# Sparse attention and a rational MLP on one core: the tensor between them stays on chip, turned, and the order of all instructions comes from a table

## The chip, the cores and the metric

One core of a Trainium2 chip runs the whole program in one launch. The metric is device time in microseconds (us). The engines are TensorE (PE in the rows, with its weight loads as PEld), VectorE (DVE), ScalarE (ACT), GpSimd (POOL) and SyncE (SP); here the last two only issue DMAs. Each engine works through its own list in order and waits on semaphores.

## The reference

Attention over 8 batches x 8 heads x 576 tokens x 64 dimensions, then an MLP over the 4608 tokens:

```
scores = q @ k.T / 8
heads 0-3 (local):   key j is seen by query i if 0 <= i-j < 32
heads 4-7 (strided): key j is seen by query i if j <= i and j % 32 == i % 32
x = softmax(masked scores) @ v          -> [4608, 512]
h = x @ w_in                            (512 -> 2048)
P = a0 + a1 h + a2 h^2 + a3 h^3
Q = 1 + |b0| |h| + |b1| h^2
out = (P / (Q + 1e-6)) @ w_out          (2048 -> 512), float32
```

The MLP needs x turned: its 512 features on the partitions, the tokens along the row.

## The kernel before

**Attention, batch by batch.** POOL issues DMAs that cast q, k, v from float32 to bf16: into DRAM scratch (`qk16`, `v16`) for batches 2 to 7, and, for batches 0 and 1, q and k into SBUF staging tiles `sg` (L441). SP then loads: for batches 2 to 7 three DMA transposes bring q and k with the head dimension on the partitions (`sqkT` L485, `lqT` and `lkT` L491); for batches 0 and 1 TensorE turns `sg` (L537) and DVE and ACT write the result out of PSUM (L553), `lqT` and `lkT` with a stride of 8 elements on the written side. The local V goes from the bf16 scratch into `vL` in 128-byte rows (L500, L508 for batches 0 and 1; L500, and L514 for the shifted copy, after that). `vS` (strided V) is cast straight into SBUF by POOL (L454).

Scores are small matmuls into PSUM (L599, L614 strided; L674 local) on top of a mask matmul (L586, L660). A row maximum (DVE L631, L698) is subtracted by a matmul (L638, L705), and ACT takes the exponential (L644, L711, L715) into `pS` and `pL`. P is turned: by TensorE and an eviction for batches 0 and 1 (L571, L578), by a DMA transpose on SP after that (L561). For the strided heads a matmul with `BO` gives the row sums (L734), DVE inverts them (L738); P is stationary and V moves (L750), two PSUM tiles of two banks one after the other, each scaled by DVE into `xS` (L757). For the local heads a column of ones in `vL` gives the sum beside P.V (L783, three banks), DVE scales into `xl` (L800, L803).

**x goes through DRAM.** `xS` and `xl` are stored in token order to `xs16` by SP: four DMAs (L765), one (L808) and two (L817) per batch. One or two DMA transposes per batch (L870, the function `gather`) bring x back turned into `xt`, a ring of three tiles of 512 tokens. For chunk 0's 512 tokens (batch 0) and the last 448 tokens of chunk 1 (batch 1) `turn_x` does it on TensorE (L836, L853) with evictions L843 and L860.

**The MLP, in 9 chunks of 512 tokens.** 16 groups of four matmuls (L889) make h in PSUM; ACT writes each out (L893). Then per group of 2 to 8 blocks of 512: |h| on ACT (L909; on DVE for chunk 0, L913), Q on DVE (L916, L918), 1/Q as exp(-ln Q) on ACT (L922, L927), P on DVE (L931 to L939), the product (L941). L957 multiplies by w_out, ACT evicts (L965), SP stores (L971).

**What sets the order.** `Prog.schedule` (L124) is a list planner: each operation carries an assumed duration and a key, `_place` (L113) gives PSUM banks (8 in all) as they come free in the plan, and the result is one fixed list per engine. `emit` (L219) adds the semaphore waits. Attention of batch b+1 is laid among the MLP of chunk b. The casts of batch b+2 wait until the loads of batch b+1 have landed.

Of the kernel before, what the change touches and what calls it, by code (L numbers as in the profile page):

```python
# [12 lines left out]
NBANK = 8  # L13
# [9 lines left out]
class Op:  # L23


    def __init__(self, eng, maker, dur, occ, key, dma, bank):
        self.eng, self.maker, self.dur, self.occ, self.key = eng, maker, dur, occ, key
        self.dma, self.bank = dma, bank
        self.dst = None
        self.gen = 0  # L30
        self.deps = {}
        self.users = []
        self.fin = None


class Tile:
# [9 lines left out]
    def new(self):  # L46
        self.prev = self.w + self.r
        self.w, self.r = [], []
        self.gen += 1
        return self  # L50


class Banks:

    def __init__(self, n):
        self.n = n
        self.ops = []
        self.w, self.r, self.prev = [], [], []  # L60
        self.at = None
        self.left = 0

    def col(self, bank=0, c=0):
        return (self.at + bank) * 512 + c


class Prog:
    ENG = ("pe", "act", "dve", "pool", "sp")

    def __init__(self, nc):
        self.nc = nc
        self.ops = []

    def op(self, eng, maker, dur, key, r=(), w=(), m=(), dma=None, occ=None, after=(), hard=()):
        bank = None
        for t in tuple(w) + tuple(m):
            if isinstance(t, Banks) and not t.ops:
                bank = t
        o = Op(eng, maker, dur, dur if occ is None else occ, key, dma, bank)  # L80
# [12 lines left out]
        o.hard = hard  # L93
# [6 lines left out]
        for t in tuple(r) + tuple(w) + tuple(m):  # L100
            if isinstance(t, Banks) and o not in t.ops:
                t.ops.append(o)
        o.banks = [t for t in dict.fromkeys(tuple(r) + tuple(w) + tuple(m)) if isinstance(t, Banks)]
        if dma is not None:
# [7 lines left out]

    def _place(self, n, t):  # L113
        rng = range(0, NBANK - n + 1) if n > 1 else range(NBANK - 1, -1, -1)
        best = None
        for i in rng:
            f = max(self.bfree[i:i + n])
            if f <= t:
                return i, f
            if best is None or f < best[1]:  # L120
                best = (i, f)
        return best

    def schedule(self):  # L124
        E = self.ENG
        for o in self.ops:
            o.ndep = len(o.deps)
            o.ready = 0.0
            for d in o.deps:
                d.users.append(o)  # L130
            for b in o.banks:
                b.left += 1
        self.bfree = [0.0] * NBANK
        self.blast = [[] for _ in range(NBANK)]
        ready = {e: [] for e in E}
        free = {e: 0.0 for e in E}
        order = {e: [] for e in E}
        qfree = {'hw': 0.0, 'sw': 0.0}
        for o in self.ops:
            if o.ndep == 0:  # L140
                ready[o.eng].append(o)
        left = len(self.ops)
        while left:
            best = None
            for e in E:
                q = ready[e]
                if not q:
                    continue
                t0 = free[e]
                pick = None  # L150
                block = False
                soon = None
                for o in sorted(q, key=lambda o: (o.key, o.idx)):
                    s = max(t0, o.ready)
                    if o.bank is not None:
                        if block:
                            continue
                        at, f = self._place(o.bank.n, s)
                        if f > s + 1e-9:
                            s = f  # L160
                            if o.bank.n > 1 and o.ready <= t0 + 1e-9:
                                block = True
                    if s <= t0 + 1e-9:
                        pick = (t0, o)
                        break
                    if s < 1e8 and (soon is None or s < soon[0] - 1e-9):
                        soon = (s, o)
                c = pick or soon
                if c is not None and (best is None or c[0] < best[0] - 1e-9):
                    best = (c[0], e, c[1])  # L170
            assert best is not None, "no bank"
            t, e, o = best
            if o.bank is not None:
                b = o.bank
                at, f = self._place(b.n, t)
                assert f <= t + 1e-6
                b.at = at
                for i in range(at, at + b.n):
                    for d in self.blast[i]:
                        o.deps.setdefault(d, 1)  # L180
                    self.bfree[i] = 1e9
            ready[e].remove(o)
            free[e] = t + o.occ
            o.start = t
            if o.dma is not None:
                us, lat = o.dma
                me, other = ("sw", "hw") if o.eng == "pool" else ("hw", "sw")
                s = max(qfree[me], t + o.dur)
                rest = max(0.0, qfree[other] - s)
                if us <= rest:  # L190
                    qfree[me] = s + 2 * us
                    qfree[other] += us
                else:
                    qfree[me] = s + us + rest
                    qfree[other] += rest
                o.fin = qfree[me] + lat
            else:
                o.fin = t + o.dur
            order[e].append(o)
            left -= 1  # L200
            for b in o.banks:
                b.left -= 1
                if b.left == 0:
                    end = [x for x in b.ops]
                    f = max(x.fin for x in end) + 0.1
                    for i in range(b.at, b.at + b.n):
                        self.blast[i] = end
                        self.bfree[i] = f
            for u in o.users:
                lat = (0.15 if o in u.hard else 0.035) if u.eng == o.eng else 0.1  # L210
                u.ready = max(u.ready, o.fin + lat)
                u.ndep -= 1
                if u.ndep == 0:
                    ready[u.eng].append(u)
        self.order = order
        self.span = max(o.fin for o in self.ops)


    def emit(self):  # L219
        nc = self.nc  # L220
        sems = {e: nc.alloc_semaphore(f"s_{e}") for e in self.ENG}
        cnt = {e: 0 for e in self.ENG}
# [15 lines left out]
        for o in self.ops:  # L238
            if o.dma is not None:
                semof[src(o)] = o.dst.sem  # L240
# [69 lines left out]
def bass_strided_sparse_attn__then__act_rational_pade_kernel(nc, q, k, v, moe_w_in, moe_w_out, moe_a, moe_b, out):  # L310
# [7 lines left out]
    CH = 512  # L318
# [725 lines left out]
```

How the kernel before makes its waits and increments, by code:

```python
            def go(eng):  # L279
                for ws, o in queues[e]:
                    for s, n in ws:
                        eng.wait_ge(s, n)
                    inst = o.maker(eng)
                    if o.dma is not None:
                        inst.then_inc(o.dst.sem, 16)
                    else:
                        inst.then_inc(sems[e], 1)
                if e == "sp":
                    for s, n in fin.items():
                        eng.wait_ge(s, n)
```

## Time and profile before

| | us |
|---|---|
| median of 3 runs | 450.33 (449.14 to 452.17) |
| span of the profiled execution, first to last instruction | 441.2 |
| what lies around the span: median less span | 9.1 |
| PE busy / DVE busy / ACT busy | 339.6 / 331.8 / 323.4 |
| DMA, hardware queue (SP) / software queue (POOL), share of 16 engines' span | 47.0% / 25.4% |
| mean granted TensorE clock (1 is 2.4 GHz) | 0.919 |

The page gives the profiled execution by its span alone, so sums are made against 441.2 us, and 9.1 us are added to compare with the runs. Three engines are each busy for about three quarters of the span: the rows have to say what they wait for, and when.

### The profile page before, as it was taken

To read this page: it belongs to the slowest core of one execution; us is meant where nothing else is said; L and a number is where in the kernel's file an instruction comes from. 1 tells how busy PE (TensorE), PEld (TensorE's weight loads), DVE (VectorE), ACT (ScalarE), POOL (GpSimd) and SP (SyncE) were. 2 spreads that over 40 slices of the span, in tenths; PEclk is the share of its full clock that TensorE was granted. 3 is DMA by queue.
4 is the path that set the end of the run, shared out by engine and by line. 5 is a ranking of instruction groups with operands and counts; after the bars stand their busy time and mean duration, and the time that the engine had idled before them with its cause. 6 is when DMAs were issued, how large, how long until landed. Compare 5 with 4: busy or idle time off the path is not lost.

```text
span 441.2 us, 10622 instructions
## 1 busy us (share of the span) xinstructions
PE 339.6 (77%) x4782; PEld 166.9 (38%) x4834; DVE 331.8 (75%) x252; ACT 323.4 (73%) x337; POOL 48.0 (11%) x80
## 2 busy tenths in 40 slices
PE   1371749895995897979868967697859999967685
PEld 0340436443442344434424433343424444423232
DVE  1632398898958579999775785859896798898991
ACT  0620487769684799897765983779858999998971
POOL 7262000005005005005002200000000000000000
PEclk9999969898897799979989968999969999996979
DMA  7999997288999999997998999332224011010012
GB/s 117 166 203 156 222 130 120 51 108 153 132 175 237 200 150 204 199 175 144 196 201 159 173 188 216 45 79 89 53 52 104 24 49 48 0 49 24 24 49 96
DMA packets 121534, 54.72 MB, mean 124 GB/s; under 512 B 101008, under 2 KB 114576, under 8 KB 120976
## 3 DMA queue, kind: packets, MB, share of 16 engines
q1 hardware_dynamic: 109520, 35.67, 47.0%
q0 software_dynamic: 11968, 18.37, 25.4%
q8 instruction: 38, 0.62, 0.6%
q14 instruction: 8, 0.07, 0.0%
HBM read 39.79 MB, written 22.61 MB: 141 GB/s over the span
## 4 chain that ended last, share of the span: by engine, by line
ACT 32%; PE 30%; DMA 12%; SPq 11%; DVE 9%; issue 5%; POOL 0%; ACTq 0%; POOLq 0%
PE ps L889 15%; ACT u L922 9%; PE ps L957 9%; ACT u L927 8%; ACT h L893 6%; ACT z L909 6%; DMA vL<-v 4%; SPq L508 4%; DMA xt<-xs 4%; SPq L500 2%; SPq L491 2%; SPq L485 2%; ACT os L965 2%; DVE u L918 2%; PE ps L783 1%
## 5 line engine op out<-in xcount | busy, mean ns | idle before, releaser
L957 PE MATMUL ps<-Wout,h 128*128 128x512 bf16 x548 | 144.9, 403 | 17.1 <-DVE h L941 7.5
L889 PE MATMUL ps<-xt,Win 128*128 128x512 bf16 x558 | 146.5, 403 | 13.1 <-DMA xt<-xs 7.9
L893 ACT ACTIVATE h<-ps 128x512 bf16<-128x512 f32 x144 | 81.5, 610 | 50.4 <-PE ps L889 50.3
L957 PEld LDWEIGHTS ps<-Wout,h 128*128 128x128 bf16 x576 | 56.0, 102 | 84.2 <-issue 15.0
L889 PEld LDWEIGHTS ps<-xt,Win 128*128 128x128 bf16 x576 | 55.8, 102 | 83.7 <-issue 12.6
L922 ACT ACTIVATE u<-u,consts 128x2048 bf16<-128x2048 bf16 (+1 forms) x40 | 71.4, 1830 | 3.2 <-DVE u L918 3.2
L927 ACT ACTIVATE u<-u 128x2048 bf16<-128x2048 bf16 (+1 forms) x40 | 67.6, 1737 | 0.1
L909 ACT ACTIVATE z<-h 128x2048 bf16<-128x2048 bf16 (+1 forms) x34 | 60.2, 1822 | 2.0 <-DVE h L941 1.7
L916 DVE TENSOR_SCALAR u<-z,coef 128x4096 bf16<-128x4096 bf16 (+2 forms) x21 | 25.1, 1195 | 25.0 <-ACT z L909 25.0
L918 DVE TENSOR_TENSOR u<-u,z 128x4096 bf16<-128x4096 bf16 (+2 forms) x21 | 41.9, 1996 | 0.6
L937 DVE TENSOR_TENSOR z<-z,h 128x4096 bf16<-128x4096 bf16 (+2 forms) x21 | 41.7, 1985 | 0.5
L933 DVE TENSOR_TENSOR z<-z,h 128x4096 bf16<-128x4096 bf16 (+2 forms) x21 | 41.6, 1983 | 0.5
L941 DVE TENSOR_TENSOR h<-z,u 128x4096 bf16<-128x4096 bf16 (+2 forms) x21 | 41.6, 1979 | 0.4
L965 ACT ACTIVATE os<-ps 128x512 f32<-128x512 f32 x36 | 21.4, 604 | 19.6 <-PE ps L957 18.5
L537 PE MATMUL ps<-IDN,sg 72*64 72x72 bf16 x256 | 8.4, 238 | 22.4 <-DMA sg<-in_q_dram 9.0
L931 DVE TENSOR_SCALAR z<-h,coef 128x4096 bf16<-128x4096 bf16 (+2 forms) x21 | 24.8, 1181 | 0.5
L431 POOL DMA_DIRECT2D qk<-in_q_dram x12 | 6.2, 516 | 174.2 <-DMA vL<-vL 174.2
L757 DVE TENSOR_TENSOR xS<-ps,rc 128x1024 bf16<-128x1024 f32 x16 | 19.3, 1220 | 7.6 <-PE ps L750 7.6
L935 DVE TENSOR_SCALAR z<-z,coef 128x4096 bf16<-128x4096 bf16 (+2 forms) x21 | 23.7, 1127 | 0.4
L939 DVE TENSOR_SCALAR z<-z,coef 128x4096 bf16<-128x4096 bf16 (+2 forms) x21 | 23.6, 1123 | 0.5
L454 POOL DMA_DIRECT2D vS<-in_v_dram x32 | 21.2, 674 | 11.6 <-PE ps L750 11.6
L750 PE MATMUL ps<-vS,ptS 18*32 18x64 bf16 x1024 | 10.9, 209 | 12.9 <-issue 8.0
(68 smaller groups left out, 234.1 us busy)
## 6 DMA issues: line engine op xcount, KB each, us to landing
out_dram<-os SPq DMA_DIRECT2D x36, 256.0 KB, 2.9
qk<-in_q_dram POOLq DMA_DIRECT2D x12, 288.0 KB, 6.7
qk<-in_k_dram POOLq DMA_DIRECT2D x12, 288.0 KB, 7.4
v<-in_v_dram POOLq DMA_DIRECT2D x8, 288.0 KB, 9.3
vS<-in_v_dram POOLq DMA_DIRECT2D x32, 72.0 KB, 10.6
vL<-v SPq DMA_DIRECT2D x32, 72.0 KB, 4.6
Win<-in_moe_w_in_dram POOLq DMA_DIRECT2D x2, 1024.0 KB, 18.9
Wout<-in_moe_w_out_dram POOLq DMA_DIRECT2D x2, 1024.0 KB, 25.2
```

What stands on the lines that cost most here:

```text
L889: r = e.matmul(bank(ph, 0, CH), Win[:, kk, f * 128:(f + 1) * 128], xt.t[:, kk, :], start=(kk == 0), stop=(kk == NK1 - 1))
L893: P.op("act", lambda e, f=f, ph=ph, h=h, f0=f0: e.activation(h.t[:, f - f0, :], bank(ph, 0, CH), AF.Copy), 0.6, ky, r=[ph], w=[h], occ=0.48)
L909: P.op("act", lambda e, z=z, h=h, i=i, hp=hp: e.activation(z.t[:, hp * i:hp * i + hp, :], h.t[:, hp * i:hp * i + hp, :], AF.Abs), dact, ky ...
L916: dv(lambda e, z=z, u=u, G_=G_: e.tensor_scalar(u.t[:, 0:G_, :], z.t[:, 0:G_, :], b1_ap, b0_ap, op0=Alu.mult, op1=Alu.add), True, 2, r=[z, ...
L918: dv(lambda e, z=z, u=u, G_=G_: e.tensor_tensor(u.t[:, 0:G_, :], u.t[:, 0:G_, :], z.t[:, 0:G_, :], op=Alu.mult), False, 4, r=[z], m=[u])
L922: lns.append(P.op("act", lambda e, u=u, i=i, hp=hp: e.activation(u.t[:, hp * i:hp * i + hp, :], u.t[:, hp * i:hp * i + hp, :], AF.Ln, bias ...
L927: exs.append(P.op("act", lambda e, u=u, i=i, hp=hp: e.activation(u.t[:, hp * i:hp * i + hp, :], u.t[:, hp * i:hp * i + hp, :], AF.Exp, sca ...
L933: dv(lambda e, z=z, h=h, G_=G_: e.tensor_tensor(z.t[:, 0:G_, :], z.t[:, 0:G_, :], h.t[:, 0:G_, :], op=Alu.mult), False, 8, r=[h], m=[z])
L937: dv(lambda e, z=z, h=h, G_=G_: e.tensor_tensor(z.t[:, 0:G_, :], z.t[:, 0:G_, :], h.t[:, 0:G_, :], op=Alu.mult), False, 11, r=[h], m=[z])
L941: dv(lambda e, z=z, h=h, u=u, G_=G_: e.tensor_tensor(h.t[:, 0:G_, :], z.t[:, 0:G_, :], u.t[:, 0:G_, :], op=Alu.mult), False, 14, r=[z, u], ...
L957: r = e.matmul(bank(po, 0, Fout), h.t[:, j, m * 128:(m + 1) * 128], Wout[:, kk, :], start=(kk == 0), stop=(kk == NF - 1))
L965: P.op("act", lambda e, o=o, po=po: e.activation(o.t[:, :], bank(po, 0, Fout), AF.Copy), 0.6, ky + m * 8 + 7, r=[po], w=[o], occ=0.48)
```

## The change

- **x stays on chip.** `XT` [128, 4, 4608] in SBUF holds all of x turned; `xs16`, its stores, `gather`, `turn_x` and the `xt` ring go. In all 8 batches: (strided) P is summed, inverted and divided on DVE before it is turned, and V is stationary with P moving, so that P.V comes out turned; two PSUM tiles of two banks are open together, and one DVE and one ACT eviction of 576 columns each write `XT`. (local) TensorE turns `xl` in ten 128-column transposes, and one DVE and one ACT eviction of 576 columns write `XT`.
- **First V as float32.** For batches 0 and 1 SP loads V without a cast, as 256-byte rows (local) and 2 KB rows (strided), into tiles that the MLP uses later; DVE and ACT cast into `vL` and `vS`. The cast of v for these batches goes from POOL's list.
- **Other first loads.** Only batch 0 is turned by TensorE from staged q and k; batch 1 goes through DRAM and DMA transposes like the rest. Batch 0's `lqT`, `lkT`, `sqkT` are written in contiguous rows.
- **Order from a table.** `_place` and `schedule` go; one list of operation numbers per engine and one digit per PSUM tile are written in the file. Mask matmuls no longer wait for the loads.

```diff
+            XT = sb("XT", [128, NK1, NT])
...
+        P.op("dve", lambda e: e.tensor_reduce(rcS.t[:, 0:32], pg(), axis=AX.X, op=Alu.add), ...
+        P.op("dve", lambda e: e.reciprocal(rcS.t[:, 0:32], rcS.t[:, 0:32]), ...
+        P.op("dve", lambda e: e.tensor_tensor(pg(), pg(), rcS.t[:, 0:32].unsqueeze(2).broadcast_to([128, 32, NI]),
...
-            P.op("pe", sav, 64 * 0.014, key, r=[ptS, vS], w=[AS])
-            P.op("dve", lambda e, AS=AS, b2=b2: e.tensor_tensor(
+        AS = [Banks(2) for _ in range(2)]
+                            r = e.matmul(bank(AS[pair], 512 * b2 + NI * (8 * odd + 2 * a + p), NI,
+                                              64 * hh, 64 * hh + 64),
+                                         vS.t[32 * bq:32 * bq + NI, h, 2 * a + p, :],
+                                         ptS.t[32 * bq:32 * bq + NI, 4 * p + h, 32 * a:32 * a + NI], ...
+            P.op(e_, evict(e_, lambda pair=pair: XT[:, 2 + pair, t0:t0 + S].rearrange(...
...
-            P.op("sp", lambda e, t=t, r0=r0, n=n, col=col: e.dma_start_transpose(
-                t.t[:, :, col:col + n], xs[b * S + r0:b * S + r0 + n, :]), 1.3, key, r=[T_xs[b]], w=[t],
+            P.op("pe", trl, "xturn", ("xtr", b, pair), r=[xl, T_id], w=[TL])
+            P.op(e_, evict(e_, lambda pair=pair: XT[:, pair, t0:t0 + S], lambda TL=TL: bankb(TL, 0, S)),
...
+    def early_v(b, st):
+                    P.op("sp", lambda e, hh=hh, pair=pair, sh=sh, t=t: e.dma_start(
+                        t.t[64 * hh + 32 - 32 * sh:64 * hh + 64 - 32 * sh, 64 * sh:NB * 64].rearrange(...
+                        bass.AP(tensor=v.tensor, offset=rows(v, b, 2 * pair + hh),
+                                ap=[[D, 32], [LB * D, NB - sh], [1, D]])), ...
+            P.op(e_, cv, "cast1152", ("vcast", b, pair), r=[t], w=[vl])
+            P.op(e_, cs, "cast1024", ("vscast", b, j), r=[t], w=[vS])
...
+ORDER = {
+    "pe": (
+        "27 25 82 29 95 31 35 33 83 39 37 84 236 96-98 86 100 93 105 103 91 113 107 114 109 108 249 119 110 "
+        "117 377 134 237-238 130 240 132 136 151 157 245 247 153 261 250-252 263 254 262 155 264 259 257 185 "
...
+    "act": (
+        "28 81 32 36 40 59 87 57 101-102 94 106 79 111 120 135 131 241 133 137 152 158 248 154 141-143 265 "
...
+    "pool": (
+        "13 22 14-16 21 23 17 24 20 19 18 122 121 123 125 124 129 128 127 126 278 282-283 276-277 281 275 280 "
...
+    "sp": (
+        "1 72 44 52 0 76-77 74 66 50 2 71 75 65 5 67 43 45 55 49 53-54 42 4 47-48 3 69 64 70 60-62 227 "
```

The numbers count operations in the order in which the code makes them: 13 to 16 stage batch 0's q and k, 17 to 20 are the weights (17 and 18 w_in), 21 to 24 batch 1's q and k casts, 42 to 55 batch 0's V loads, 56 to 59 its V casts, 60 to 62 batch 1's DMA transposes, 64 to 77 batch 1's V loads, 78 to 81 its V casts, 83 and 84 batch 0's strided scores, 111, 112, 118 and 120 batch 0's evictions into `XT`, 121 to 129 batch 2's casts, 130 to 137 the first four w_in groups with their evictions, 236 to 238 batch 1's strided mask and scores, 377 batch 2's strided mask.

## Rows read from the trace of the kernel before

**Rows 1.** Stretches: length; busy us of PE, PEld, DVE, ACT, POOL; clock; DMA share; GB/s.
```profile
0.00:49.50 49.50, 17.65 (x587) 13.60 (x590) 18.38 (x23) 13.87 (x13) 19.79 (x35) 1.00 1.35 166
49.50:100.00 50.50, 40.79 (x825) 23.11 (x831) 41.88 (x41) 36.56 (x45) 0.20 (x1) 0.90 0.81 116
100.00:283.00 183.00, 150.18 (x2359) 71.25 (x2385) 143.70 (x98) 140.48 (x142) 28.01 (x45) 0.90 1.02 177
283.00:340.00 57.00, 47.02 (x654) 22.45 (x663) 44.54 (x31) 44.51 (x49) 0.00 (x0) 0.91 0.31 76
340.00:400.00 60.00, 52.70 (x239) 23.27 (x243) 53.02 (x30) 59.97 (x60) 0.00 (x0) 0.98 0.09 31
400.00:441.20 41.20, 31.29 (x125) 13.19 (x126) 30.24 (x32) 28.00 (x33) 0.00 (x0) 0.87 0.14 52
```

**Rows 2.** Chain of waits, whole span: start, us, what.
```profile
28.53 14.66 DMA vL<-v
...
45.76 2.40 ACT xt L860 x2
...
134.96 8.36 DMA xt<-xs
...
266.82 4.28 DMA xt<-xs
```

**Rows 3.** Timeline of ACT: three evictions of h and the idle time before each.
```profile
145.29 0.60 ACT L893 ACTIVATE h<-ps 128x512 bf16<-128x512 f32 x1 [4.88 <-PE ps L889]
...
226.77 0.60 ACT L893 ACTIVATE h<-ps 128x512 bf16<-128x512 f32 x1 [2.73 <-PE ps L889]
...
273.08 0.60 ACT L893 ACTIVATE h<-ps 128x512 bf16<-128x512 f32 x1 [3.63 <-PE ps L889]
```

**Rows 4.** Waits of PE: waiter, releaser, us in total, times, longest.
```profile
PE ps L889 <- DMA xt<-xs: 7.9, 3, 3.5
...
PE ps L783 <- DVE z L937: 5.5, 1, 5.5
PE ps L660 <- ACT h L893: 4.5, 2, 2.2
PE ps L734 <- DMA ptS<-pS: 3.7, 2, 2.6
```

**Rows 5.** DMA queues (packets, MB, share): 0 to 50, 15 to 20, 60 to 65, 70 to 75 us.
```profile
q0 software_dynamic: 7258, 7.45, 101.4%
...
q0 software_dynamic: 595, 0.69, 108.9%
q1 hardware_dynamic: 593, 0.07, 55.6%
...
q1 hardware_dynamic: 2900, 0.36, 134.4%
...
q1 hardware_dynamic: 3640, 0.92, 115.2%
```

**Rows 6.** Groups by form: out<-in, shapes, count | busy us, mean ns | idle before.
```profile
L553 ACT ACTIVATE lqT<-ps 128x576 bf16<-128x576 bf16 x2 | 5.4, 2712 | 0.6 <-PE ps L537 0.5
...
L553 ACT ACTIVATE sqkT<-ps 128x576 bf16<-128x576 bf16 x4 | 2.6, 644 | 1.8 <-PE ps L537 1.8
...
L860 ACT ACTIVATE xt<-ps 128x224 bf16<-128x224 bf16 x2 | 2.2, 1343 | 0.3 <-PE ps L853 0.3
...
L757 DVE TENSOR_TENSOR xS<-ps,rc 128x1024 bf16<-128x1024 f32 x16 | 19.3, 1220 | 7.6 <-PE ps L750 7.6
...
L631 DVE TENSOR_REDUCE ng<-ps 128x32 bf16<-128x576 f32 x8 | 6.0, 755 | 3.5 <-PE ps L599 2.3 <-PE ps L614 1.2
...
L836 PE MATMUL ps<-IDN,xl 128*128 128x128 bf16 x16 | 1.6, 265 | 0.0
...
L909 ACT ACTIVATE z<-h 128x1024 bf16<-128x1024 bf16 x4 | 4.2, 1058 | 1.8 <-DVE h L941 1.7
```

**Rows 7.** DMA queue of SP from 283 to 297 us, x's way through DRAM.
```profile
q1 hardware_dynamic: 2470, 0.88, 28.4%
```

More of the change, by code:

```diff
@@ L73, in __init__, with op @@
         self.ops = []
[L75 to L80, printed above, removed]
+        self.banks = []
+    def op(self, eng, maker, kind, lab, r=(), w=(), m=(), dma=None, after=(), hard=()):
+        o = Op(eng, maker, kind, lab, dma)
         o.idx = len(self.ops)
@@ L110, in op @@
         return o
[L113 to L179, printed above, removed]
-                        o.deps.setdefault(d, 1)
[L181 to L216, printed above, removed]
@@ new lines, in place @@
+    def place(self, order, at):
+        self.order = {e: [self.ops[i] for i in order[e]] for e in self.ENG}
+        assert sorted(i for e in self.ENG for i in order[e]) == list(range(len(self.ops)))
+        last = [None] * 8
+        for b, a in zip(self.banks, at):
+            b.at = a
+        for o in self.order["pe"]:
+            b = o.bank
+            if b is None:
+                continue
+            for i in range(b.at, b.at + b.n):
+                if last[i] is not None:
+                    for d in last[i].ops:
+                        o.deps.setdefault(d, 1)
+                last[i] = b
@@ L264, in emit @@
                                 kn[a] = b
-                        kn[s] = max(kn.get(s, 0), d.cnt)
+                        kn[d.src] = max(kn.get(d.src, 0), d.cnt)
                     o.know = dict(kn)
-                    queues[e].append(([(semof[s], n) for s, n in need.items()], o))
-                    done.add(o)
+                    queues[e].append((list(need.values()), o))
+                    done[o] = len(done)
                     ptr[e] += 1
@@ L271, in emit @@
             assert moved, "order is cyclic"
+        used = set()
+        for o in self.ops:
+            used.update(o.deps)
         fin = {}
         for o in self.ops:
-            if o.dma is not None and not o.users:
-                fin[o.dst.sem] = max(fin.get(o.dst.sem, 0), o.cnt)
+            if o.dma is not None and o not in used:
+                fin[o.sem] = max(fin.get(o.sem, 0), o.cnt)
         def run(e):
@@ L345, in bass_strided_sparse_attn__then__act_rational_pade_kernel @@
     T_v = [Tile(f"v{b}") for b in range(B)]
-    T_xs = [Tile(f"xs{b}") for b in range(B)]
     Win = sb("Win", [128, NK1, Fmid])
@@ L980, in bass_strided_sparse_attn__then__act_rational_pade_kernel @@
+    hw = Fmid // 2
+    for i in range(2):
+        weights(i, Win[:, :, i * hw:(i + 1) * hw], w_in[:, i * hw:(i + 1) * hw], T_win, "win")
+    for i in range(2):
+        weights(i, Wout[:, 8 * i:8 * i + 8, :], w_out[1024 * i:1024 * i + 1024, :], T_wout, "wout")
+    sts[1] = casts(1)
+    loads(0, sts[0])
     nxt = 0
     for b in range(B):
-        cur = st
-        if b == 0:
-            weights_out(0, -70)
-            weights_out(1, -69)
-        key = b * PER - 26
-        if b + 1 < B:
-            st = loads(b + 1, key + 12, vS[b + 1])
@@ L989, in bass_strided_sparse_attn__then__act_rational_pade_kernel @@
-        xl, xb = attention(b, cur, key, b < NPE)
-        if b + 2 < B:
-            vS[b + 2] = casts(b + 2, key + 14, after=st["lk"].w + st["sqk"].w + st["vl"].w if b + 1 >= NPE else ())
-        if b < NPE:
-            turn_x(b, xl, xb, key + 14)
-            gather(b, key + 20, CH - b * (S - CH))
-        else:
-            gather(b, key + 18)
+        if b + 1 < B:
+            loads(b + 1, sts[b + 1])
+        attention(b, sts[b])
+        if b == 3:
+            for bb in range(4, B):
+                for t in T_x[bb]:
+                    t.new(*early)
@@ L1007, in bass_strided_sparse_attn__then__act_rational_pade_kernel, with _expand @@
+def _expand(text):
+    for part in text.split():
+        a, _, b = part.partition("-")
+        yield from range(int(a), int(b or a) + 1)
+def bass_strided_sparse_attn__then__act_rational_pade_kernel(nc, q, k, v, moe_w_in, moe_w_out, moe_a, moe_b, out):
+    P = graph(nc, q, k, v, moe_w_in, moe_w_out, moe_a, moe_b, out)
+    P.place({e: list(_expand(t)) for e, t in ORDER.items()}, [int(x) for x in AT])
     first = P.order["act"][0]
```

615 lines of the change are left out of this document (293 added, 322 removed), and 48 rows, old and new, of the table ORDER.

## The prediction

> **What bounds the kernel now.** I read the busy time by stretch first [rows 1]. Up to 49.5 us the MLP has not begun. From 340 us on there is no attention left: ACT is busy 59.97 of 60 us, so the MLP alone is bound by ACT. Between 100 and 283 us ACT works 140.5 of 183 us, PE 150.2, DVE 143.7: no engine is the bound there, each waits for the others. The idle time of ACT after 49.5 us is what a change can win: 391.7 us less 309.5 us of work (36.56 + 140.48 + 44.51 + 59.97 + 28.00) is 82.2 us. By stretch it is 13.9, 42.5, 12.5, 0 and 13.2 us.
>
> Two things are to be seen in that table. The DMA share is 1.02 from 100 to 283 us, so the transfers are then as dense as they get. But from 283 to 340 us it is 0.31, and ACT still idles 22% of the stretch, against 23% before. So the transfers are not the whole cause; the other part is attention's chain of small steps in engines that work in order.
>
> Then the chain of waits [rows 2]: it begins with the last local V load of batch 0, which lands at 43.2 us, and reaches the first w_in matmul at 49.5 us by P.V, the turning of x and slow evictions. Later it holds x's way back from DRAM, 8.36 us at 135 and 4.28 us at 267 us. ACT's timeline has the cost: right after these gathers, and after a third at 222 us, ACT waits 4.88, 2.73 and 3.63 us for PE [rows 3], which waits for x [rows 4]. That is 11.2 us of the 82.2.
>
> So the time is written as T = S + W + I: the start S of the MLP (49.5), ACT's work after it (309.5), its idle time after it (82.2). The profiled span is 441.2 us; the median of the runs is 9.1 us more, and I add that at the end.
>
> **S, the start.** The chunk's first matmul needs all of batch 0's x. The last evictions into `XT` on ACT stand behind the cast of batch 1's V (79 before 111 and 120), so they need every V load of both batches: 2 x 4480 rows of 256 bytes and 2 x 288 rows of 2 KB, 9536 packets on SP's queue, against 4480 of 128 bytes before 49.5 us now. How fast do they come? From 15 to 20 us POOL's queue moved 595 packets and SP's 593 [rows 5]: while both have work, SP's queue gets one packet for each of POOL's. With POOL's queue empty it moved 2900 in 5 us, and 3640 of larger ones. POOL's first transfers are eight casts of 288 KB and four weight halves of 1024 KB, 6.4 MB; at 7.45 MB in 50 us that is 43 us, with 7258 x 6.4 / 7.45 = 6235 packets, so SP's queue has as many by then. The other 3301 take 4.5 us at 3640 in 5 us. Batch 2's casts join in by then; I add 2 us: 50 us. The last cast is about 1.06 us (an ACT operation of 1024 bf16 columns [rows 6]), two evictions 2 x 0.64, hand-overs about 1: S = 54, 4.5 later than now. Bounds: 31 if the V loads are not held back by POOL's queue (w_in's first half then decides: 3.04 MB before it, 20 us, and some 10 us of attention), 62 if batch 2's casts (1.7 MB, 11 us) hold them one for one too.
>
> The Trainium skill speaks against such small pieces: "DMA: Bandwidth & Descriptors", section Specifications, wants at least 512 bytes a transfer for line rate. The rows agree only in part: the larger packets came more often in 5 us, not less [rows 5]. By the page's fabric ceiling of 435 GB/s, an estimate, the 3.5 MB would take 8 us.
>
> **W, ACT's work.** Gone after S: batch 1's turned q and k, 2 x 2.71 + 2 x 0.64 = 6.7 us, and its turned x, 2.2 us [rows 6]. New: two evictions in each of seven batches. Their price isn't in the trace; the nearest are 576 columns at 0.644 us and, written with a stride, 224 columns at 1.343 us. Local x is written in rows, strided x in rows from strided reads, as the 0.644 was; I take 0.644 for both, 9.0 us, and keep 13.9 as the upper end. W = 309.5 - 6.7 - 2.2 + 9.0 = 309.6. Batch 0's cheaper evictions and the V casts lie before S, under the wait for V.
>
> **The other engines.** DVE loses 2 x 1.220 us per batch (scaling `xS`) and gains a sum (0.755 from the nearest row, the maximum of 576), a product of 576 (0.75 likewise), two evictions (2 x 0.64) and a small inversion in place of one like it: +0.35 us per batch. DVE is idle 39 us from 100 to 283 us [rows 1]; covered, and if that is gone it costs 3 us in all. PE gains 64 transposes at 0.1 us, 6.4 us [rows 6], and loses batch 1's 128 turning matmuls, the sums and `turn_x`: taken as even, within 4 us. P.V keeps its count of matmuls. SP loses nine issues per batch. POOL loses ten casts of V; batch 2's casts now wait for batch 0's strided scores, with only later casts behind them.
>
> **I, the idle time.** (a) x's three waits go: -11.2. What is late next in that place is attention of the following batch; it has its own waits, left in. (b) In the 13.9 us from 49.5 to 100 us the turning of batch 1 (evictions of 2.71 us before PE may go on) is the larger part, say 7. In its place PE's list has batch 1's strided scores (237, 238) as second step after one w_in group; they wait for a DMA transpose that SP issues behind all V loads. All w_in groups queue behind this wait, and ACT behind them. I take 3 us of it as not covered: -4. (c) Per batch SP and the DMA engines lose x's stores and gather. From 283 to 297 us, where little else moved, SP's queue took 28.4% of 14 us, 4.0 us [rows 7], so about a tenth of a 36 us batch. The DMA transposes of P, for which PE waits 3.7 us by itself [rows 4] and ACT behind it longer, get issued earlier: -6, between 0 and -10. (d) The order itself: unknown; 0 here, a rival below. I = 82.2 - 11.2 - 4 - 6 = 61.
>
> **Sum.** T = 54 + 309.6 + 61 = 424.6 us, and 433.7 with what lies around the span: **434 us**, 3.6% less. From the bounds without the far one of S: S 47 to 62, W up to +5, I within 9: 420 to 446.
>
> **Rivals.**
> - *The order closes attention's own waits as well.* PE waits 5.5 us at L783 and 4.5 at L660 [rows 4] not for data but for its turn or for PSUM banks. If ACT's 55 us of idle time between 100 and 340 us fall to 17 instead of 38, T is 21 less: 413. For: most of it isn't transfers. Against: the same chain of steps remains, longer by three DVE steps before P is turned. 422 us, 0.24.
> - *V is not held back.* S = 31, T = 402, 411 us. Against: 595 to 593 [rows 5]. 0.03. The page's ceiling above would give this.
> - *x's wait gives way to another.* From 283 to 340 us ACT idles as much without dense transfers. If (a) and (c) bring nothing, I is 78, T = 54 + 309.6 + 78 = 442, 451 us: no change. 0.12.
> - *PSUM banks: slower.* The strided P.V holds four banks at once instead of two and two, batch 2's mask takes two before the first w_in groups, the local P.V three: of eight, one to three are left for the MLP, and w_in groups wait for evictions. The nearest price is the 5.5 us wait of L783, which now occurs once; in five more batches it is 27.5 us: T = 452, 461 us. It decides from 3 us a batch on. Against: the digits of the table can keep the pairs apart. 0.13.
>
> **How the numbers follow.** The forecast has 0.48. What a measurement can tell here from no change is 1%: 445.8 to 454.8 us. Faster: 0.48 + 0.24 + 0.03 = 0.75; same 0.12; slower 0.13. The range takes the forecast's 420 to 446, goes down to 411 for the first two rivals and up to 453 for the third; about 0.1 is left out on either side.
>
> **What would show it.** S: the first w_in matmul near 54 us, its releaser an `XT` eviction on ACT behind a V cast; SP's and POOL's packet counts equal up to 43 us. W: ACT's busy time after S near 310 us, evictions into `XT` near 0.65 us. I: no wait of PE for x after the start; DMA share from 100 to 283 us near 0.9; ACT's idle time there nearer to 30 us than to 42. Wrong would be: S beyond 62 us, or w_in matmuls that wait for evictions of h in every batch, or ACT 77% busy as now.

## The result, and the profile after

The changed kernel takes 422.22 us (median of 4 runs, 420.45 to 424.48) against 451.25 us for the kernel before, run beside it: ratio 0.937, 95% interval 0.931 to 0.943, so 6.3% faster. Some executions of a kernel come out slower than others; the ratios and their intervals leave these out, the medians don't. The forecast was 434 us, 3.6% less. The range held the time, but the terms of the sum were off by up to 27 us, in opposite directions. This is the changed kernel by stretch (length; busy us of PE, PEld, DVE, ACT, POOL; clock; DMA share; GB/s), from its first w_in matmul on, with the columns of [rows 1]:

```profile
0.00:75.40 75.40, 19.77 (x572) 13.36 (x572) 17.50 (x32) 12.44 (x16) 12.24 (x23) 1.00 1.05 188
75.40:100.00 24.60, 21.15 (x439) 10.77 (x438) 17.55 (x21) 16.95 (x25) 6.70 (x12) 0.86 0.88 122
100.00:283.00 183.00, 167.13 (x2532) 80.73 (x2531) 160.58 (x121) 166.11 (x177) 24.78 (x36) 0.97 0.74 134
283.00:340.00 57.00, 55.19 (x837) 26.48 (x835) 53.66 (x39) 57.00 (x60) 0.00 (x0) 1.00 0.49 74
340.00:400.00 60.00, 51.83 (x231) 22.31 (x230) 57.69 (x36) 59.05 (x61) 0.00 (x0) 0.94 0.08 31
400.00:419.90 19.90, 15.29 (x71) 6.76 (x69) 11.97 (x19) 11.59 (x17) 0.00 (x0) 1.00 0.32 119
```

By the forecast's own terms, T = S + W + I of the profiled span:

| | before | forecast | after |
|---|---|---|---|
| S, start of the MLP | 49.5 | 54 | 75.4 |
| W, ACT's work after it | 309.5 | 309.6 | 310.7 |
| I, ACT's idle time after it | 82.2 | 61 | 33.8 |
| span | 441.2 | 424.6 | 419.9 |
| around the span | 9.1 | 9.1 | 1.8 |

The columns show 21 of the 29 us between the medians: the profiled execution of the kernel before took 441.2 + 1.8 = 443 us and is quicker than every timed one on record (444.1 and more), so a usual one has some 7 us more in S, W or I than the column says.

The MLP starts 26 us later than before, and the kernel is faster all the same, since ACT hardly waits after that: from 100 to 283 us it idles 16.9 us (before 42.5), from 283 to 340 us not at all (before 12.5).

**What starts the MLP so late.** The chain of waits of the changed kernel (start, us, what; SPq is SP issuing a DMA). The pieces from 8 to 43 us are SP's issues too, of V loads and, in between, of a mask (5.41 us at 9.0) and a load of coefficients (4.07 us at 24.3):

```profile
43.79 9.41 SPq L392
...
53.24 6.92 DMA z<-in_v_dram
...
60.19 0.69 DVE vS L413
60.88 0.67 DVE ng L561
...
62.22 1.26 DVE ng L640
...
65.38 1.74 PE ps L501 x13
...
70.50 0.66 ACT XT L452
...
73.44 0.66 ACT XT L452
...
75.47 1.84 PE ps L764 x4
```

One of SP's loads of V takes 9.41 us to be issued, the one behind it, the last of batch 0's strided V, lands at 60.2 us, and only then does batch 0's softmax begin: `ng` (L561) is the row maximum of its strided scores. The timeline of PE says how long the scores had been ready:

```profile
61.61 0.66 PE L568 MATMUL ps<-ng,IDN 128*128 128x288 bf16 x2 [16.44 <-DVE ng L561]
```

PE has stood there for 16.44 us. The maximum needs no V: it stands behind the cast of V on DVE, because the table has the cast (58) ahead of it (85). And why the load was late is in the DMA queues of the changed kernel (packets, MB, share), from 25 to 30, 50 to 55 and 60 to 65 us:

```profile
q0 software_dynamic: 619, 0.78, 87.8%
q1 hardware_dynamic: 621, 0.25, 27.8%
...
q0 software_dynamic: 84, 0.68, 64.5%
q1 hardware_dynamic: 85, 0.05, 3.5%
...
q1 hardware_dynamic: 3567, 0.86, 100.0%
```

From 15 to 40 us SP's queue (q1) moves one packet for each of POOL's (q0), as in [rows 5]. From 50 to 55 us POOL's are packets of 8 KB (0.68 MB in 84) and SP's queue gets 85 packets through in 5 us; with POOL's queue empty it moves 3567. Those 8 KB packets are batch 2's casts, which POOL issued at 43.7 to 46.2 us. That 84 and 85 are equal is chance, as shorter stretches show, 46 to 48 and 50 to 52 us:

```profile
q0 software_dynamic: 63, 0.31, 76.3%
q1 hardware_dynamic: 476, 0.19, 37.1%
...
q0 software_dynamic: 42, 0.39, 91.3%
q1 hardware_dynamic: 20, 0.01, 2.5%
```

So after 40 us the counts are not one for one, in either direction; why, these views don't say. That the casts hold SP's queue is tested below (casts_of_2_later).

**What else answers to the rows of before.** No wait of PE for x is left after the start ([rows 4] had 7.9 us). The evictions into `XT`, forecast at 0.644 us by [rows 6], by form:

```profile
L452 DVE CAST XT<-ps 128x576 bf16<-128x576 f32 x8 | 6.0, 752 | 3.4 <-PE ps L678 3.4
...
L452 ACT ACTIVATE XT<-ps 128x576 bf16<-128x576 bf16 x8 | 5.5, 683 | 2.4 <-PE ps L741 2.3
L452 ACT ACTIVATE XT<-ps 128x576 bf16<-128x576 f32 x8 | 5.5, 683 | 4.1 <-PE ps L678 4.1
```

**One change more.** |h| moves too. Before, DVE makes it for all three groups of chunk 0 (L913); in the changed kernel ACT makes it for the second and the third (the table `MLP`, `[0, 1, 1]`), four operations more on ACT. The forms of |h| on ACT, before (its other form, x4, is in [rows 6]) and after:

```profile
L909 ACT ACTIVATE z<-h 128x2048 bf16<-128x2048 bf16 x30 | 56.0, 1924 | 0.2
```
```profile
L784 ACT ACTIVATE z<-h 128x2048 bf16<-128x2048 bf16 x32 | 63.0, 2006 | 0.1
...
L784 ACT ACTIVATE z<-h 128x1024 bf16<-128x1024 bf16 x6 | 6.4, 1152 | 0.0
```

### The profile page after: what moved, and what is told of

The parts are those of the page before. It is cut to its first block, busy times and chain, and to the rows that moved or that the text cites. A ratio compares the mean times of both kernels' runs of the same rounds, so it can differ in the third digit from the quotient of the medians.

```text
span 419.9 us, 10298 instructions
## 1 busy us (share of the span) xinstructions
PE 330.4 (79%) x4674; PEld 160.4 (38%) x4674; DVE 318.9 (76%) x266; ACT 323.1 (77%) x351; POOL 43.7 (10%) x70
## 4 chain that ended last, share of the span: by engine, by line
ACT 42%; PE 25%; DVE 11%; SPq 11%; DMA 7%; issue 4%; ACTq 0%
PE ps L833 12%; ACT z L784 10%; ACT u L798 9%; ACT h L768 9%; ACT u L803 9%; PE ps L764 8%; SPq L382 4%; SPq L392 4%; DVE u L794 4%; DMA out_dram<-os 3%; DMA ptL<-pL 2%; DVE u L791 2%; ACT os L841 2%; DMA z<-in_v_dram 2%; SPq L294 1%
## 5 line engine op out<-in xcount | busy, mean ns | idle before, releaser
L833 PE MATMUL ps<-Wout,h 128*128 128x512 bf16 x576 | 138.9, 387 | 8.6 <-DVE h L818 7.5
L764 PE MATMUL ps<-XT,Win 128*128 128x512 bf16 x576 | 137.6, 385 | 5.1 <-ACT h L768 2.6
L833 PEld LDWEIGHTS ps<-Wout,h 128*128 128x128 bf16 x576 | 54.6, 99 | 73.9 <-DVE h L818 8.4
L764 PEld LDWEIGHTS ps<-XT,Win 128*128 128x128 bf16 x576 | 54.2, 99 | 73.8 <-ACT h L768 8.2
L803 ACT ACTIVATE u<-u 128x2048 bf16<-128x2048 bf16 (+1 forms) x40 | 72.1, 1817 | 0.1
L784 ACT ACTIVATE z<-h 128x2048 bf16<-128x2048 bf16 (+1 forms) x38 | 69.4, 1871 | 0.2
L351 POOL DMA_DIRECT2D vS<-in_v_dram x24 | 18.0, 751 | 71.5 <-PE ps L833 41.4
L320 POOL DMA_DIRECT2D qk<-in_k_dram x14 | 7.1, 510 | 134.8 <-DMA vL<-vL 100.8
L678 PE MATMUL ps<-ptS,vS 18*64 18x18 bf16 x1024 | 14.4, 183 | 7.0 <-issue 2.7
L512 PE MATMUL ps<-MS,IDN 128*128 128x288 bf16 x16 | 4.3, 361 | 18.5 <-DMA M<-c 16.7
L678 PEld LDWEIGHTS ps<-ptS,vS 18*64 18x64 bf16 x1024 | 12.0, 119 | 13.9 <-issue 5.9
```

The source lines that it names most:

```text
L764: r = e.matmul(bank(ph, 0, CH), Win[:, kk, f * 128:(f + 1) * 128], XT[:, kk, c * CH:c * CH + CH], start=(kk == 0), stop=(kk == NK1 - 1))
L784: P.op("act", lambda e, z=z, h=h, i=i, hp=hp: e.activation(z.t[:, hp * i:hp * i + hp, :], h.t[:, hp * i:hp * i + hp, :], AF.Abs), f"act_{h ...
L803: exs.append(P.op("act", lambda e, u=u, i=i, hp=hp: e.activation(u.t[:, hp * i:hp * i + hp, :], u.t[:, hp * i:hp * i + hp, :], AF.Exp, sca ...
L833: r = e.matmul(bank(po, 0, Fout), h.t[:, j, m * 128:(m + 1) * 128], Wout[:, kk, :], start=(kk == 0), stop=(kk == NF - 1))
```

## The experiments

The change has three parts that can each be the cause: x's way through DRAM goes, the operations are others, the order is others. The runs below take them apart, then go after the start, then after what x's traffic costs. S, W and I are read from the profile of each run; ratios are to the kernel before, run on the same chip.

| kernel | median us | ratio (95%) | span | S | W | I |
|---|---|---|---|---|---|---|
| changed kernel | 422.22 | 0.937 (0.931 to 0.943) | 419.9 | 75.4 | 310.7 | 33.8 |
| nox_planner | 439.43 | 0.970 (0.954 to 0.986) | 431.0 | 49.4 | 309.5 | 72.1 |
| after_planner | 448.06 | 1.001 (0.993 to 1.009) | 446.1 | 67.4 | 315.0 | 63.7 |
| after_planner_dma | 491.23 | 1.078 (1.070 to 1.086) | 484.0 | | | |
| head_casts_later | 421.34 | 0.940 (0.933 to 0.948) | 418.6 | 73.3 | 310.8 | 34.6 |
| head_reordered | 422.63 | 0.942 (0.932 to 0.952) | 416.8 | 48.6 | 312.7 | 55.5 |
| head_reordered_2 | 404.75 | 0.896 (0.888 to 0.903) | 402.5 | 46.7 | 312.5 | 43.3 |
| head_reordered_3 | 404.66 | 0.903 (0.893 to 0.913) | 404.4 | 48.6 | 312.5 | 43.3 |
| casts_of_2_later | 416.50 | 0.929 (0.917 to 0.940) | 415.7 | 68.3 | 310.9 | 36.5 |
| table_with_dead_traffic | 450.40 | 0.982 (0.974 to 0.990) | | | | |
| table_with_dead_stores | 434.95 | 0.972 (0.960 to 0.983) | 432.8 | 73.3 | 311.1 | 48.4 |
| dead_stores_casts_later | 430.61 | 0.954 (0.945 to 0.963) | 428.5 | 73.9 | 310.9 | 43.8 |
| after_casts_5_later | 426.99 | 0.944 (0.933 to 0.955) | 426.9 | 74.4 | 310.8 | 41.7 |

A row of this table comes from one view, the busy time after S; of the changed kernel, for instance (the third busy time from the right is ACT's, 344.50 - 310.70 = 33.8):

```profile
75.40:419.90 344.50, 310.59 (x4103) 147.05 (x4102) 301.45 (x234) 310.70 (x335) 31.48 (x48) 0.97 0.57 104
```

### Which part of the change gains

**nox_planner**: the kernel before without x's way through DRAM. Its planner stays. Every chunk reads chunk 0's x (so the output is not x's), and waits for the attention that makes its own.

```diff
-        for a in range(4):
-            P.op("sp", lambda e, a=a: e.dma_start(bass.AP(tensor=xs, ...
...
-            P.op("sp", lambda e, t=t, r0=r0, n=n, col=col: e.dma_start_transpose(
...
-        xt = xt_of[c]
+        xt = xt_of[0]
+        after_x = [] if c == 0 else [o for b in range(B) if ... for o in made[b]]
```

> The kernel before without x's way through DRAM: its stores (L765, L808, L813, L817) and its gathers (L870) are left out. All MLP chunks read chunk 0's turned x (so the output is not the reference's), and chunk c still waits for the last DVE scaling of the batches that it would read, so that order and dependencies stay. The planner is the old one. Theory X (x's way through DRAM cost the time): 11 us of waits for x and some 6 us for queues go, ratio to the kernel before 0.955 to 0.97. Theory O (the order of the lists costs the time, x was in the way only because of where it stood): another wait takes the place, ratio 0.98 to 1.0.

Measured: 3.0% less (1.4 to 4.6), at the edge of theory X's range; I from 82.2 to 72.1. Taking x's stores and gathers away gives 10 us of idle time in the old order, where the forecast had -11.2 and -6 for (a) and (c).

**after_planner**: the changed kernel's operations, put in order by the planner of before (its durations, keys and assumed DMA times); masks wait for the loads again.

```diff
-    P.place({e: list(_expand(t)) for e, t in ORDER.items()}, [int(x) for x in AT])
+    P.place(*P.schedule())
```

> The changed kernel's operations in an order made by the list planner of the kernel before, with the old durations, keys and DMA assumptions, in place of the table; mask matmuls wait for the loads again. x stays on chip, V is float32 first. Theory X: most of the gain stays, ratio to the kernel before 0.93 to 0.955. Theory O: the gain goes, ratio 0.98 to 1.03, and ACT idles over 40 us between 100 and 340 us.

Measured: no gain at all. I is 63.7, almost the forecast's 61, but S is 67.4 and W 315.0. So without the table the change gives back at the start what it wins later. With the table I is 33.8: **the table is worth 30 us of idle time** on these operations, and it costs 8 us at the start. The table is the order, the places in PSUM and the masks that don't wait; this run changes the three together, and no run gives such a table to the operations of before. Where these 30 us lie is in the waits of ACT for w_in results (us in total, times, longest), in the kernel before, in this one and in the changed one:

```profile
ACT h L893 <- PE ps L889: 50.3, 46, 4.9
```
```profile
ACT h L950 <- PE ps L946: 36.7, 43, 3.6
```
```profile
ACT h L768 <- PE ps L764: 10.9, 17, 3.2
```

Each has 144 such evictions. With the planner's list ACT comes 43 times before the matmuls are done, with the table 17 times; that is 25.8 of the 30 us. TensorE's granted clock goes with the list: over the span it is 0.889 with the planner and 0.971 with the table (1 is 2.4 GHz), and the same matmuls keep PE busy for 346.3 and 330.4 us. Part of the 30 us can therefore be PE's slower work; how large a part, and what in the planner's list lowers the clock, no run here separates.

**after_planner_dma**: the same planner, told longer DMA times.

```diff
-    return d, c, key, dma
+    return d, c, key, (o.dma, 2.0) if o.dma is not None else None
```

> As the changed kernel in the old planner's order, but the planner is told the longer DMA times that the changed file carries (7.2 us for the strided transpose instead of 2.6, 3.6 for the local ones, 1.0 per V load instead of 0.47, and so on); engine durations as before. Theory D (the old order is bad because it takes transfers for shorter than they are): most of the table's gain comes back, ratio to the kernel before 0.94 to 0.97. Rival S (it is the rule of always taking the most urgent ready operation, with any durations): ratio 0.98 to 1.02.

Measured: 8% slower, outside both theories' ranges. That the table is only what the planner would give with better DMA times falls; what the table knows in their place these runs don't tell.

### The start

**head_casts_later**: batch 0's V casts behind its maximum, sums and exponentials in DVE's and ACT's lists.

```diff
-  dve "... 26 80 30 34 38 58 85 56 99 88 6 89-90 78 104 92 ..."
+  dve "... 26 80 30 34 38 85 99 88 6 89-90 58 56 78 104 92 ..."
-  act "28 81 32 36 40 59 87 57 101-102 94 106 79 111 ..."
+  act "28 81 32 36 40 87 101-102 59 57 94 106 79 111 ..."
```

> The changed kernel with two edits in its lists: on DVE the casts of batch 0's V (58, 56) stand behind batch 0's maxima and P's division (85 to 90), on ACT 59 and 57 behind the exponentials. Theory L (in-order lists hold batch 0's softmax behind V's landing at 60 us): P is ready when V lands, the first w_in matmul comes at 67 to 69 us instead of 75.5, the time falls by 6 to 9 us to 413 to 416. Theory V (the landing of V alone sets the start, the softmax is hidden under it): within 2 us of 422.

Measured: 2 us earlier, no gain that can be told from none. Another operation takes the casts' place: 6 on DVE, which waits for the MLP's coefficients, still stands ahead of the division of P (89, 90), and SP issues the coefficients behind V loads. In this run DVE waits 13.39 us, until 61.5 us, for the last of them (`consts`). PE's timeline:

```profile
62.77 0.61 PE L501 MATMUL ps<-IDN,pS 128*128 128x128 bf16 x4 [14.13 <-DVE pS L585]
```

**head_reordered**: all first lists (SP's is shown): SP issues constants, then batch 0's V, then the rest; DVE takes 6 and batch 1's V casts behind batch 0's attention, ACT its V casts of batch 1 behind the first w_in groups; POOL casts batch 1's q and k ahead of w_out, and w_out comes behind batch 2's casts.

```diff
-  sp "1 72 44 52 0 76-77 74 66 50 2 71 75 65 5 67 43 45 55 49 ..."
+  sp "0-2 52-55 42-45 47-50 5 4 3 60-62 74-77 64-67 69-72 227 ..."
```

> The changed kernel with the heads of four lists rewritten, the rest and the PSUM places kept: SP issues the constants, then batch 0's V, then batch 1's DMA transposes, then batch 1's V; POOL issues batch 0's q and k, the first w_in half, batch 1's casts, the second w_in half, then (after batch 0's strided P.V) batch 2's casts and w_out; DVE and ACT take batch 1's V casts after the first w_in groups. Theory L with Q (SP's queue gets one packet per packet of POOL's, so the order of issue decides when batch 0's V lands): V lands near 33 us, first w_in matmul at 38 to 46 us, time 385 to 400 us, if the rest of the table holds. Rival R (the rest of the table is laid for a start at 75 us; batch 1 or w_out come late and the idle time returns): 405 to 422 us.

Measured: the first w_in matmul at 48.6 us, 27 us earlier, and the time unchanged, at the upper end of its rival's range: I grows by 22 us. The late V is now batch 1's, and in DVE's list its cast stands ahead of batch 1's maximum, as batch 0's did before. DVE's and PE's timelines of this kernel:

```profile
70.40 0.77 DVE L404 CAST vL<-z 128x1152 bf16<-128x1152 f32 x1 [15.04 <-DMA z<-in_v_dram]
```
```profile
71.88 0.66 PE L568 MATMUL ps<-ng,IDN 128*128 128x288 bf16 x2 [19.21 <-DVE ng L561]
```

**casts_of_2_later**: the changed kernel, and POOL's casts of batch 2 wait for batch 1's V as well. Nothing else differs.

```diff
-  casts(b + 2, after=... else sts[b]["sqk"].r)
+  casts(b + 2, after=... else sts[b]["sqk"].r + sts[1]["vl"].w + sts[1]["vS"].w)
```

> The changed kernel with one dependence more: POOL's casts of batch 2 also wait for batch 1's V casts from float32. Lists and all else as in the changed kernel. Theory A (bulk transfers of POOL's queue hold SP's queue packet for packet: from 50 to 55 us 84 packets of POOL's to 85 of SP's): the last V load lands near 52 us instead of 60.2, the first w_in matmul comes at 65 to 69 us instead of 75.4, and the time falls by 4 to 8 us, to 414 to 418 us. Theory B (SP's queue is late by its own many small packets, not by POOL's): last V load at 59 to 61 us, first w_in matmul at 74 to 77 us, 420 to 425 us.

Measured: the last load of batch 0's strided V lands at 53.1 us instead of 60.2, the first w_in matmul comes at 68.3 instead of 75.4, and the time is 416.5 us, 5.7 less (415.3 to 417.5, below every run of the changed kernel; the intervals of the two ratios, 0.929 and 0.937, overlap). The chain of waits of this kernel (start, us, what), and SP's queue from 50 to 55 us, where POOL's is now empty:

```profile
37.87 6.38 SPq L382
...
45.47 7.61 DMA z<-in_v_dram
53.10 0.69 DVE vS L413
```
```profile
q1 hardware_dynamic: 2930, 0.82, 80.2%
```

So batch 2's casts held SP's queue, 85 packets in that stretch for 2930, and 7 of S's 21 us too many are theirs.

**head_reordered_2**: head_reordered with that dependence, the same correction for batch 1 on DVE (239, its maximum, ahead of 80 and 78), and SP issuing batch 1's `lqT` and `lkT` behind its V.

```diff
-  dve "... 6 80 78 239 ..."
+  dve "... 6 239 80 78 ..."
-  sp "0-2 52-55 42-45 47-50 5 4 3 60-62 74-77 64-67 69-72 227 ..."
+  sp "0-2 52-55 42-45 47-50 60 5 4 3 69-72 74-77 64-67 61-62 227 ..."
```

> The changed kernel with the heads of its lists rewritten a second time: SP issues constants, batch 0's V, batch 1's strided transpose, coefficients, batch 1's V, then batch 1's local transposes; DVE takes batch 1's strided maximum before batch 1's V casts (in the last one it stood behind them and PE waited 19 us for it); batch 2's casts and w_out on POOL also wait until batch 1's V has been cast. Theory L with Q: the first w_in matmul at 46 to 50 us and no wait above 4 us on PE after it, so the 25 us that the start is earlier show at the end: 392 to 402 us. Rival R (the rest of the table is laid for a start at 75 us): 408 to 420 us, with new waits of ACT between 80 and 200 us.

Measured: 404.75 us, 10.4% less than the kernel before and faster than the changed kernel (the intervals of the two ratios don't touch), but between its two theories' ranges. It is the fastest version here, beside head_reordered_3. What is late next is w_out, held behind batch 2's casts: a wait of more than the 4 us that were expected at most. PE's timeline:

```profile
79.22 1.87 PE L833 MATMUL ps<-Wout,h 128*128 128x512 bf16 x4 [6.19 <-DMA Wout<-in_moe_w_out_dram]
```

**head_reordered_3**: the first half of w_out ahead of batch 2's q and k, and ACT's casts of batch 1's V, for which POOL's casts of batch 2 wait (POOL's gate), earlier.

```diff
-  act "... 120 135 131 241 133 137 79 81 152 ..."
+  act "... 120 135 131 79 81 241 133 137 152 ..."
-  pool "... 18 129 128 127 126 122 121 123 125 124 19 20 278 ..."
+  pool "... 18 129 128 127 126 19 122 121 123 125 124 20 278 ..."
```

> The kernel of head_reordered_2 with ACT's two casts of batch 1's V four steps earlier (they open POOL's gate) and the first half of w_out ahead of batch 2's remaining casts. Theory A (what is left of the start is w_out, which landed at 79.2 us there): w_out's first half lands at 64 to 70 us, no wait of more than 2 us for it, first w_in matmul at 45 to 49 us, 395 to 401 us. Rival (batch 2's casts come late in its place, PE and ACT wait for batch 2's turned q and k between 75 and 110 us): 403 to 408 us. Lost if ACT's earlier casts hold batch 0's evictions: first w_in matmul beyond 50 us.

Measured: the wait for w_out is gone, the time is the same (404.66). The gate opened at 56.1 us instead of 56.9, hardly earlier. In head_reordered_2 and here ACT is busy for 15.3 and 23.2 us between 75 and 100 us, so the wait's 8 us are won there; it loses 5.1 us before 75 us, where PE waits 5.5 us at 62 us (2.25 in head_reordered_2) for nothing that the profile shows, and 4.8 between 100 and 130 us, where ACT waits 6.22 us before 122 us for w_in results. The rival had the size right and the place, turned q and k, wrong.

### What x's traffic costs under the table

**table_with_dead_traffic**: the changed kernel, with x's old stores and gathers as transfers that nobody reads, in batches 2 to 6.

```diff
+    for b in range(2, B - 1):
+        for a_ in range(4):
+            P.op("sp", lambda e, a_=a_, t0=t0: e.dma_start(bass.AP(tensor=xs, ...), Win[...]), ...
+        ...
+            got.append(P.op("sp", lambda e, ...: e.dma_start_transpose(XT[:, :, NT - S + r0:...], xs[...]), ...
```

> The changed kernel with x's old transfers put back as dead ones for batches 2 to 6: SP issues the same seven stores (from a constant tile) and two gathers (into the place of batch 7's x, not read before batch 7 overwrites it) at about the old places of its list; nothing waits for them but SP itself. If SP's queue and the DMA engines were what x's way cost: 5 to 10 us more than the changed kernel (427 to 432 us). If only the wait for x cost: within 3 us of 422.

Measured: 4.8% above the changed kernel by the two ratios (0.982 to 0.937), some 20 us, though nobody waits for this x; that is far above both expectations. Its profile is not read here; the next run stands in for it.

**table_with_dead_stores**: the same without the gathers, seven stores a batch.

> The changed kernel with x's old stores to DRAM as dead transfers in batches 2 to 6, seven issues a batch at the places where table_with_dead_traffic had them, without its gathers. With both, the time was 4.8% above the changed kernel, some 20 us. Theory A (the gathers cost, as DMA transposes of 3 to 4 us in SP's queue ahead of P's): stores alone cost under 1.2%, 420 to 427 us. Theory B (the stores cost, by seven issues a batch and their packets): 433 to 445 us. Both by half: 428 to 433 us.

Measured: 434.95 us, 12.7 above the changed kernel, 3.7% by the ratios against 4.8% with the gathers; so the stores make the larger part of the price, and since the intervals of those two ratios overlap, what the gathers add isn't shown. ACT's idle time is 48.4 us, 14.6 more, and 12.64 of the 48.4 are one wait (4.37 in the changed kernel). The chain of waits, and PE's and ACT's timelines:

```profile
196.91 17.75 DMA ptL<-pL
```
```profile
214.70 0.68 PE L709 MATMUL ps<-vL,ptL 64*32 64x65 bf16 x36 [10.60 <-DMA ptL<-pL]
```
```profile
219.12 0.60 ACT L841 ACTIVATE os<-ps 128x512 f32<-128x512 f32 x1 [12.64 <-PE ps L833]
```

The transpose of batch 4's local P, issued at 196.9 us, takes 17.75 us (10.18 in the changed kernel), and PE's whole list stands behind it. It runs beside batch 5's casts; POOL's queue has work from 200 to 205 and still from 205 to 210 us, where in the changed kernel only 4 packets of it are left:

```profile
q0 software_dynamic: 206, 0.57, 121.1%
q1 hardware_dynamic: 478, 0.13, 26.9%
...
q0 software_dynamic: 145, 0.41, 42.3%
q1 hardware_dynamic: 278, 0.07, 16.4%
```

**dead_stores_casts_later** and **after_casts_5_later**: batch 5's casts wait for that transpose, with the dead stores and without.

```diff
+    pt = [o for o in P.ops if o.lab == ("pturn", 4, "L")]
+    for o in P.ops:
+        if o.lab[:2] == ("cast", 5):
+            o.deps[pt[0]] = 1
```

> The kernel of table_with_dead_stores (434.95 us, ACT's idle time after the start 48.4 us) with one dependence more: POOL's casts of batch 5, at 194 to 201 us there, also wait for the DMA transpose of batch 4's local P, for which PE waited 10.6 us. Theory A (the stores cost because they make this transpose late enough to run one for one against the casts): that wait is below 2 us, ACT's wait of 12.6 us behind it goes, 424 to 428 us. Theory B (the stores cost by SP's issues and packets wherever they stand; batch 5's later casts give the wait back): 432 to 438 us.

> The changed kernel with the same dependence: batch 5's casts also wait for the DMA transpose of batch 4's local P, for which PE waited 2.9 and ACT 4.4 us. Theory A: both waits go, 417 to 420 us. Theory B (batch 5's turned q and k come later by as much): 421 to 425 us.

Measured: 430.61 and 426.99 us, 4.3 less with the stores and 4.8 more without (the runs of the latter, 423.5 to 428.8, overlap those of the changed kernel by 1 us, and the ratios' intervals overlap too, so the 4.8 are not clear of noise). The wait for `ptL` is gone in both, and another stands in its place. SP's queue and PE's timeline of the kernel without stores:

```profile
207.12 6.84 SPq L429 DMA_TRANSPOSE lqT<-qk  x1
214.01 1.31 SPq L491 DMA_TRANSPOSE ptS<-pS  x1
```
```profile
217.57 0.60 PE L678 MATMUL ps<-ptS,vS 18*64 18x18 bf16 x32 [7.67 <-DMA ptS<-pS]
```

SP's list has batch 5's `lqT` ahead of batch 4's `ptS`. The casts that `lqT` needs come later, so P's strided half waits in its turn. Neither theory is right as put: the wait for `ptL` goes, as theory A has it, and the time follows in part with the stores and not without. With this dependence the stores cost 3.6 us (ratios 0.954 and 0.944, intervals overlapping), without it 12.7 (0.972 and 0.937, intervals apart). So their price depends on what stands beside them.

## Why the prediction was right, point by point

**The total was right because two errors cancelled.** S came out 21.4 us over the forecast, W 1.1 over, I 27.2 under: -4.7 in all on the span. The time fell 7 us further below the forecast for the fourth term, what lies around the span. The prediction's own sign of being wrong, S beyond 62 us, came.

**S, 54 forecast, 75.4 measured: failed.** Three things in it. (1) The one-for-one counts came true from 15 to 40 us (432 to 437, 621 to 619, 708 to 710). But by 43 us POOL's queue had moved 4650 packets and SP's 5233, where the forecast had 6235 for both, since it took over the packets of the kernel before, of 1.0 KB; here POOL's are of 1.3 KB. Then it let batch 2's casts take 2 us and kept 11 us as the far bound (62); casts_of_2_later shows 7. The rule was not applied to its end: SP's rate is POOL's rate in packets, and larger packets of POOL's make it smaller. The Trainium skill, "DMA: Bandwidth & Descriptors", section "Queues, rings and completion order", has each DMA engine go round the queues that have work, a packet from each. The equal counts up to 40 us agree with it, and so do 190 to 187 at 5.3 KB (head_reordered, 20 to 25 us); 476 to 63 and 20 to 42 after that, in counts over all 16 engines, don't show it. (2) After the last V load that counts the forecast had a cast, two evictions and hand-overs, 4 us. Measured are 15.2 us from the landing of batch 0's strided V: batch 0's maximum, exponentials, division, turning, P.V and turning of x, all in series, since the table put casts of V ahead of the maximum. The prediction looked for such a cast ahead of the evictions (79 before 111 and 120) and not further up the same lists. (3) head_casts_later shows that this is not one cast: with it moved, the coefficients hold the same place.

**W, 309.6 forecast, 310.7 measured: right in size, in part by luck.** The evictions on ACT took 0.683 us each for the 0.644 taken. The four operations of |h| that moved to ACT are missing from the sum; at the means of before (1.924 and 1.058 us) they are 6 us, and W should have come to 316. What can have made up for them is overlap between ACT's operations: after S the busy times of its groups add up to 347.7 us for 310.7 of busy time, before to 326.4 for 309.5. In after_planner, with more gaps, W is 315.0, 2.2 of it casts of V.

**I, 61 forecast, 33.8 measured: failed, in the other direction.** The term that failed is (d), "The order itself: unknown; 0 here": it was set at nothing without a reason. With the old planner the same operations leave 63.7, 3 from the forecast; the table leaves 33.8. (a) and (c) together measured -10 in the old order for -17. Their price depends on the order: under the table the stores alone cost 3.6 or 12.7 us, by what stands beside them. The prediction also read a DMA share of 1.02 as transfers as dense as they get, where [rows 1] has 1.35 before 49.5 us; from 100 to 283 us the share is now 0.74, for the 0.9 forecast. (b), -4, no run takes apart. The rival "The order closes attention's own waits as well" is what happened: from 100 to 340 us ACT idles 16.9 us, where it said 17. Its time of 422 us was added wrongly, though: 433.7 less 21 is 413 with the 9.1 us already in it. That it agrees with the result is chance; S, 21 us late, made up for it. How the range's 420 and 446 follow from the parts is not worked out either; the 47 us for S have no row.

**The other rivals.** "V is not held back": no. "x's wait gives way to another": with the planner's order, yes in time (448 us), but by S, not by I. "PSUM banks": no; w_in matmuls wait 2.6 us in all for evictions of h.

**The 9.1 us around the span: failed.** They were the median of before less the span of one execution. The changed kernel's profiled run took 421.72 us for a span of 419.9, so 1.8 us lie around it. With as much around it, the profiled execution of the kernel before took 443 us, 7 less than its median; it was one of its quicker ones. That is 7 us of the forecast's excess of 12.

**A later start is partly paid back.** From the changed kernel to head_reordered_2, S falls by 28.7 us and the span by 17.4: I rises from 33.8 to 43.3. 9.7 us of it now lie between 75 and 100 us, where PE waits 6.19 us for w_out. In the changed kernel w_out is issued at 7 to 8 us and lands within 35 us, long before S.

## What to carry to other kernels

When lists are fixed and in order, read each list up from the instruction that the forecast names, to its head: any cast or constant that waits for a DMA and stands ahead of the critical operation can move the whole start. Where two DMA queues share the engines, ask in packets, not in bytes: a few bulk transfers can hold a queue of small packets (85 in 5 us here, 2930 without them), so try holding the bulk back until the small ones have landed, and look at what waits for the bulk. And don't set an unknown order at nothing: run the new operations under the old planner to see what the order is worth.

## What the runs showed of the hardware

SP's queue moved 85 packets in 5 us beside 84 of 8 KB, 621 beside 619 of 1.3 KB, and 3567 with nothing beside it; with the 8 KB packets held back, 2930 in the same 5 us (casts_of_2_later). At the changed kernel's start equal counts hold from 15 to 40 us, and not from there to 54 us (476 to 63, 20 to 42). One issue of a DMA on SP took up to 9.41 us in such a stretch, so that constants behind it in SP's list were late as well: the last load of constants was issued at 57.8 us.
